# Two chained MLPs on one core: the last product's rows streamed over activations held as weights

## The chip, the cores and the metric

The kernel runs on one core of a Trainium2 chip. The metric is the device time of one execution in microseconds, and lower is better. Every time below was taken before the change.

## The reference

```python
B, S, D = 2, 4096, 192                # x; 8192 tokens in all, 8 heads of 24 features, 7 taps
w = softmax(weight_gen, axis=-1)      # (B, S, 8, 7), with 1e-9 added to the sum
x_unf = causal_windows(x, 7)          # each token and its 6 predecessors
x = einsum('bshk,bskhg->bshg', w, x_unf).reshape(8192, 192)

h = maximum(x @ w_in1, 0)             # w_in1 (192, 2048)
x = (h * h) @ w_out1                  # w_out1 (2048, 192)

h = x @ w_in2                         # w_in2 (192, 2048)
g = h * clip(h + 3, 0, 6) / 6
return g @ w_out2                     # w_out2 (2048, 192), result (8192, 192) float32
```

Four matrix products follow the small convolution: two for layer one, two for layer two. The change is to the last of them, `g @ w_out2`.

## The kernel before, in words

**Precision.** Every float32 operand of a product is split into a high part, rounded to the format fp32r, and a low part, the rest. A product is then high times high, plus high times low, plus low times high.

**Tokens.** The 8192 tokens are taken in 16 chunks of 512 (`CHUNKS`, `N`). Token rows are dealt so that partition p holds 64 consecutive rows, and a chunk is four of them in each of 128 partitions (`J = 4`).

**Steps.** The 2048 inner features are 16 tiles of 128, taken two at a time (`PAIR`), so that each layer of each chunk has 8 steps (`STEPS`) and the kernel has 256. In a step g TensorE makes the first product of step g into the bank pair `h_ps[:, s % 2]` and the second product of the step two before it (`LAG = 2`), from `hid_hi` and `hid_lo`, into `y1_ps` (layer one) or `y2_ps` (layer two). Between them ScalarE applies relu (L458), VectorE squares or gates (L820, L822), ScalarE rounds to the high part (L503) and VectorE takes the low part (L831), each over 128x1024 elements.

**Two halves of the array.** All these matmuls use 64 of the array's 128 rows: the upper half (partitions 64 to 127) and the lower half (0 to 63) run as two tiles side by side, on different PSUM banks. Each matmul has its own load of 128 weight columns, and the program alternates between the halves. One half of one step's first product is 9 matmuls of 512 columns (`hidden_part`, L1131). One half of one step's second product is 10 matmuls of 512 columns: six for the first 128 output features (`main_part`, L1141) and four for the other 64, whose high and low weights stand side by side in one 128-wide load (`rest_part`, L1149). So a step is 19 matmuls of 512 columns on each half. In each of them the output matrix is the weight and the 512 tokens are streamed, so the sums stand as features by tokens. `head`, `first_body` and `second_body` write out the order: in the first body the upper half makes the step's first product while the lower half finishes the second product; in the second body the roles are changed.

**The output.** Since the sums stand as features by tokens, ScalarE copies them out of PSUM with the factor 1/6 (`copy_o`, L552 and L553), VectorE adds the cross sum (`add_o`, L861) and turns 32x32 blocks (`turn_out`, L754 and L755), and the SP queue stores them in 32 small DMAs for each chunk (`store_turned`, L368 and L377). The last chunk is turned on TensorE instead (`turn_last_out`, L1291 and L1296) and stored by one DMA (L382).

**The last steps.** `last_bodies` and `output_sums` make the last chunk's sums; the last two steps' products use the full 128 rows of the array (L1253 to L1263).

**What sets the order.** Each engine's program is written out by hand, and engines wait on counting semaphores. TensorE waits, besides others, for `hi_done` and `lo_done` (the high and low inner activations of a step), and for its own `main_upper`, `main_lower`, `rest_upper` and `mm2_done`, which keep the two halves from adding into the same bank at once.

Of the kernel before, what the change touches and what calls it, by code (L numbers as in the profile page):

```python
# [18 lines left out]
def conv_mlp_kernel(nc: bass.Bass, x: bass.AP, weight_gen: bass.AP, w_in1: bass.AP, w_out1: bass.AP,  # L19
# [12 lines left out]
    P = 128  # L32
# [18 lines left out]
    HI_REST, LO_REST = slice(P, D), slice(D, D + REST)  # L51

# [52 lines left out]
    out_blocks = out.rearrange("(b t r) (f q) -> f t b r q", b=PBLOCKS, t=Q, q=Q)  # L105
# [5 lines left out]
    with ctx:  # L111
# [35 lines left out]
        o_main, o_rest, o_cross = outs[:, 0:N], outs[:, N:N + HALF], outs[0:REST, 2 * N:3 * N]  # L147
        out_sb = outs[:, 3 * N:3 * N + J * D].rearrange("p (a b d) -> p a b d", a=2, b=J // 2)
        out_main, out_rest = outs[:, 3 * N:4 * N], outs[:, 4 * N:4 * N + HALF]
# [63 lines left out]
        o_copied = sem("o_copied")  # L213
        o_added = sem("o_added")
# [3 lines left out]
        out_turned = sem("out_turned")  # L218
        last_turned = sem("last_turned")
# [20 lines left out]
        def low(n):  # L240

            layer, (kind, part, rest) = n // PIECES, PIECE[n % PIECES]
            hi, raw, _ = piece(n)
            if kind == "in":
                return [(win[layer][:, 2 * rest + 1, part * QC:(part + 1) * QC], raw, hi)]
            w = wout[layer][:, part * PT:(part + 1) * PT, :]
            return [(w[:, :, LO_MAIN], raw[:, :, 0:P], w[:, :, HI_MAIN]), (w[:, :, LO_REST], raw[:, :, P:D], w[:, :, HI_REST])]
# [71 lines left out]
        def _(sp):  # L319
# [31 lines left out]
            def store_turned(c):  # L351

                main = out_main.rearrange("p (n q) -> p n q", q=Q)
                rest = out_rest.rearrange("p (n q) -> p n q", q=Q)
                row_first = isinstance(c, int) and c < VECTOR

                def target(f, row):
                    return out_blocks[f][:, :, bass.ds(c * J + row, 1), :].rearrange("t b r q -> t b (r q)")

                def columns(blocks_of, row):  # L360
                    if row_first:
                        return blocks_of[:, row * PBLOCKS:(row + 1) * PBLOCKS, :]
                    return blocks_of.rearrange("p (b r) q -> p r b q", r=J)[:, row]

                sp.wait_ge(out_turned, 2 * c + 1)
                for f in range(P // Q):
                    for row in range(J):
                        sp.dma_start(target(f, row), columns(main[f * Q:(f + 1) * Q], row)).then_inc(out_stored, 16)  # L368
                sp.wait_ge(out_turned, 2 * c + 2)
                for half in range(2):  # L370
                    for f in range(REST // Q):
                        p0 = half * REST + f * Q
                        for n in range(J):

                            row, b0 = (half * JHALF + n // 2, n % 2 * 2) if row_first else (n, half * 2)
                            src = rest[p0:p0 + Q, 2 * n:2 * n + 2, :] if row_first else columns(rest[p0:p0 + Q], n)
                            sp.dma_start(target(P // Q + f, row)[:, b0:b0 + 2], src).then_inc(out_stored, 16)  # L377

            def store_last(c):
                sp.wait_ge(out_copied, 1)  # L380
                sp.wait_ge(out_scaled, 1)
                sp.dma_start(out_rows[:, bass.ds(c * (J * D), J * D)],  # L382
                             out_sb[:, :, :, :].rearrange("p a b d -> p (a b d)")).then_inc(out_stored, 16)
# [21 lines left out]
            def iteration(i):  # L405
                sp.wait_ge(exp_done, i + 2)
                load_gates(i + 2)
                move_blocks(i + 1)
                load_window(i + 2)
                store_turned(i - 2)  # L410
# [6 lines left out]
            for c in range(CHUNKS - 4, CHUNKS - 1):  # L417
                store_turned(c)
            store_last(CHUNKS - 1)
            sp.wait_ge(out_stored, STORES * (CHUNKS - 1) + 16)  # L420
# [19 lines left out]
        def _(act):  # L440
# [72 lines left out]
            def split_moved_hi(c, dst, free):  # L513
# [3 lines left out]
                act.activation(dst[:, 0, :], xs_main, ACT.Copy).then_inc(x1_hi, 1)  # L517
                act.wait_ge(x_rest_moved, 16 * (c - (VECTOR - 1)))
                act.activation(dst[REST:P, 3, :], xs_rest, ACT.Copy).then_inc(x1_hi, 1)
# [21 lines left out]
            def copy_o(c, steps, ps, final=0):  # L541

                act.wait_ge(mm2_done, steps)
                if not isinstance(c, int) or c >= 1:
                    act.wait_ge(out_turned, 2 * c)
                    act.wait_ge(out_stored, STORES * c)
                if final:
                    act.activation(row_major(o_cross), by_row(ps[REST:P, 1, :]), ACT.Copy).then_inc(o_copied, 1)
                    act.wait_ge(mm2_done, steps + 1)
                    act.activation(row_major(o_main), by_row(ps[:, 0, :]), ACT.Copy).then_inc(o_copied, 1)  # L550
                else:
                    act.activation(o_main[:, :], ps[:, 0, :], ACT.Copy, scale=1.0 / 6.0).then_inc(o_copied, 1)  # L552
                    act.activation(o_cross[:, :], ps[REST:P, 1, :], ACT.Copy, scale=1.0 / 6.0).then_inc(o_copied, 1)  # L553

            def copy_lower_out(c):

                act.wait_ge(last_turned, 1)
                act.wait_ge(out_stored, STORES * c)
                act.activation(out_sb[:, :, :, 0:REST].rearrange("p a b q -> p (a b) q"),
                               y2_ps[:, 0, 0:HALF].rearrange("p (j q) -> p j q", j=J), ACT.Copy, scale=1.0 / 6.0)  # L560
                act.activation(out_sb[:, 0, :, P:D], y2_ps[:, 0, HALF:2 * D].rearrange("p (b q) -> p b q", b=JHALF),
                               ACT.Copy, scale=1.0 / 6.0).then_inc(out_copied, 1)
# [79 lines left out]
            copy_o(CHUNKS - 1, g0 + STEPS, y1_ps, final=1)  # L642
            copy_lower_out(CHUNKS - 1)
# [3 lines left out]
        def _(dve):  # L647
# [103 lines left out]
            def turn_out(c):  # L751
                dve.wait_ge(o_copied, 2 * c + 2)
                dve.wait_ge(o_added, c + 1)
                dve.transpose(out_main, o_main).then_inc(out_turned, 1)  # L754
                dve.transpose(out_rest, o_rest).then_inc(out_turned, 1)  # L755

# [51 lines left out]
            def split_moved_lo(c, dst):  # L808
                dve.wait_ge(x1_hi, 2 * c + 2)
                dve.tensor_tensor(dst[:, 1, :], xs_main, dst[:, 0, :].bitcast(fp32), ALU.subtract).then_inc(x1_lo, 1)  # L810
                dve.wait_ge(x1_hi, 2 * c + 3)
                dve.tensor_tensor(dst[REST:P, 2, :], xs_rest, dst[REST:P, 3, :].bitcast(fp32),
# [39 lines left out]
            def add_o(c, ps, final=0):  # L852
                dve.wait_ge(o_copied, 2 * c + 2 - final)
                for half, rows in enumerate((slice(0, REST), slice(REST, P))):
                    if final:
                        js = slice(half * JHALF, (half + 1) * JHALF)
                        ins = dve.tensor_tensor(o_rest[rows, :].rearrange("p (j b i) -> p j b i", j=JHALF, i=Q),
                                                by_row(ps[0:REST, 1, :])[:, js], row_major(o_cross)[:, js], ALU.add)
                    else:
                        cols = slice(half * HALF, (half + 1) * HALF)  # L860
                        ins = dve.scalar_tensor_tensor(out=o_rest[rows, :], in0=ps[0:REST, 1, cols], scalar=1.0 / 6.0,  # L861
                                                       in1=o_cross[:, cols], op0=ALU.mult, op1=ALU.add)
                ins.then_inc(o_added, 1)

            def iteration(i, prep, last):
                g0 = first_step(i) if isinstance(i, int) else dve.snap(i * (2 * STEPS) - STEPS)
                for s in range(2 * STEPS):
# [11 lines left out]
                    if s == 12:  # L879
                        turn_out(i - 2)  # L880
# [3 lines left out]
                    if s == 2:  # L884
                        add_o(i - 2, y2_ps)
# [69 lines left out]
            for s in range(STEPS):  # L955
                gate(g0 + s, 1, s % 2)
                hidden_lo(g0 + s, s % 2, own=s - (STEPS - 2) if s >= STEPS - 2 else None)
                if s == 2:
                    add_o(CHUNKS - 2, y2_ps)
                if s == 3:  # L960
                    turn_out(CHUNKS - 2)
            add_o(CHUNKS - 1, y1_ps, final=1)
            dve.wait_ge(last_turned, 1)
            dve.wait_ge(out_stored, STORES * (CHUNKS - 1))
            dve.tensor_scalar(out_sb[:, :, :, REST:P].rearrange("p a b q -> p (a b) q"),
                              y2_ps[:, 1, 0:HALF].rearrange("p (j q) -> p j q", j=J), 1.0 / 6.0, None, ALU.mult)
            dve.tensor_scalar(out_sb[:, 1, :, P:D], y2_ps[:, 1, HALF:2 * D].rearrange("p (b q) -> p b q", b=JHALF), 1.0 / 6.0,
                              None, ALU.mult).then_inc(out_scaled, 1)
# [3 lines left out]
        def _(pe):  # L972
# [179 lines left out]

            def head(g, late, rest_of):

# [263 lines left out]
```

## Time and profile before

| what | value |
|---|---|
| median of 3 runs | 1126.98 us (1126.95 to 1127.29) |
| profiled execution, span of core 0 | 1125.2 us |
| TensorE matmuls busy | 1119.4 us (99%), 9940 instructions |
| TensorE weight loads busy | 1082.5 us (96%), 9940 instructions |
| VectorE busy | 906.8 us (81%) |
| ScalarE busy | 668.8 us (59%) |
| granted TensorE clock | 1.00 throughout |
| DMA packets | 79302, of which 56172 are under 512 B |

The profiled execution is a run of its own; its own time is known by its span alone, from the first instruction to the last, and the runs' times hold what lies around such a span as well. Matmuls are pipelined and their rows overlap: a row's duration is longer than the distance to the next matmul of the same half, so how fast TensorE works is read from the distances between starts.

### The profile page before, as it was taken

The page shows a single profiled execution, that of the slowest core. Times are in us where ns is not written, and L with a number is a line of the kernel's source. Part 1 is how long each engine was busy: PE and PEld are TensorE (multiplying, and loading weights), DVE is VectorE, ACT ScalarE, POOL GpSimd, SP SyncE. Part 2 cuts the span into 40 slices and gives each one's busy share as a digit, 9 for nine tenths or more (in the row PEclk, how much of TensorE's full clock was granted, in tenths as well). Part 3 has the DMA queues.
Part 4 walks back from the last instruction along what each step waited for, and adds up shares of the span by engine and source line. Part 5 has one row for each costly group of instructions (what it writes and reads, how often), then busy time and mean ns, then how long its engine had stood idle before and what let it go on. Part 6 is the DMA issues. An engine that isn't in the chain of part 4 may idle for free.

```text
span 1125.2 us, 25509 instructions
## 1 busy us (share of the span) xinstructions
PE 1119.4 (99%) x9940; PEld 1082.5 (96%) x9940; DVE 906.8 (81%) x985; ACT 668.8 (59%) x747; POOL 3.1 (0%) x10
## 2 busy tenths in 40 slices
PE   9999999999999999999999999999999999999998
PEld 8998999999999999999999999999999999999997
DVE  8788796987969789697887978879698797976665
ACT  7986556565565655645556555555655556456554
POOL 1000000000000000000000000000000000000000
PEclk9999999999999999999999999999999999999999
DMA  7221002020110201103020020200202002010001
GB/s 214 86 66 36 6 16 63 4 74 7 30 48 3 75 6 57 25 0 77 4 66 15 0 77 4 70 11 8 69 4 73 8 17 59 0 40 4 1 16 29
DMA packets 79302, 41.28 MB, mean 37 GB/s; under 512 B 56172, under 2 KB 72300, under 8 KB 79272
## 3 DMA queue, kind: packets, MB, share of 16 engines
q1 hardware_dynamic: 79144, 40.64, 13.9%
q8 instruction: 21, 0.34, 0.1%
q10 hardware_dynamic: 128, 0.22, 0.1%
q14 instruction: 9, 0.07, 0.0%
HBM read 29.42 MB, written 11.40 MB: 36 GB/s over the span
## 4 chain that ended last, share of the span: by engine, by line
PE 99%; DVE 0%; DMA 0%; ACT 0%; issue 0%; DVEq 0%
PE h_ps L1131 46%; PE y_ps L1141 31%; PE y_ps L1149 21%; PE h_ps L988 0%; DMA wraw<-in_weight_gen_dram 0%; PE y_ps L1099 0%; PE y_ps L988 0%; PE y_ps L1272 0%; PE h_ps L1099 0%; PE y_ps L1253 0%; DVE prod L721 0%; PE y_ps L1254 0%; PE y_ps L1259 0%; PE y_ps L1256 0%; PE h_ps L1089 0%
## 5 line engine op out<-in xcount | busy, mean ns | idle before, releaser
L1131 PE MATMUL h_ps<-xt,win 64*128 64x512 f32 x4552 | 1026.4, 386 | 0.0
L1131 PEld LDWEIGHTS h_ps<-xt,win 64*128 64x128 f32 x4552 | 801.3, 184 | 14.9
L1141 PE MATMUL y_ps<-hid_hi,wout 64*128 64x512 f32 x2032 | 542.5, 386 | 0.0
L503 ACT ACTIVATE hid_hi<-hid 128x1024 fp32r<-128x1024 f32 x240 | 254.7, 1061 | 328.9 <-DVE hid L822 166.0
L831 DVE TENSOR_TENSOR hid_lo<-hid,hid_hi 128x1024 fp32r<-128x1024 f32 x253 | 309.5, 1223 | 147.6 <-ACT hid_hi L503 141.5
L1141 PEld LDWEIGHTS y_ps<-hid_hi,wout 64*128 64x128 f32 x2032 | 373.3, 184 | 7.1 <-PE y_ps L1141 0.3
L1141 PE MATMUL y_ps<-hid_lo,wout 64*128 64x512 f32 x1016 | 311.6, 386 | 0.0
L1149 PE MATMUL y_ps<-hid_hi,wout 64*128 64x512 f32 x1016 | 311.4, 386 | 0.0
L1149 PE MATMUL y_ps<-hid_lo,wout 64*128 64x512 f32 x1016 | 311.3, 386 | 0.0
L1141 PEld LDWEIGHTS y_ps<-hid_lo,wout 64*128 64x128 f32 x1016 | 186.8, 184 | 4.0 <-DVE hid_lo L806 0.3
L1149 PEld LDWEIGHTS y_ps<-hid_hi,wout 64*128 64x128 f32 x1016 | 186.9, 184 | 3.7 <-PE y_ps L1149 0.3
L1149 PEld LDWEIGHTS y_ps<-hid_lo,wout 64*128 64x128 f32 x1016 | 186.9, 184 | 3.4
L822 DVE SCALAR_TENSOR_TENSOR hid<-hid,h_ps 128x1024 f32<-128x1024 f32 x128 | 155.8, 1217 | 31.4 <-ACT hid L458 31.1
L458 ACT ACTIVATE hid<-h_ps,three 128x1024 f32<-128x1024 f32 x128 | 142.8, 1115 | 62.7 <-PE h_ps L1131 60.4
L458 ACT ACTIVATE hid<-h_ps 128x1024 f32<-128x1024 f32 x126 | 129.0, 1024 | 45.2 <-PE h_ps L1131 44.8
L820 DVE TENSOR_TENSOR hid<-hid 128x1024 f32<-128x1024 f32 x114 | 139.5, 1223 | 18.4 <-ACT hid L458 17.5
L657 DVE TENSOR_TENSOR acc<-acc,prod 128x768 f32<-128x768 f32 x84 | 80.1, 954 | 0.6
L670 DVE TENSOR_TENSOR prod<-xwin,prob 128x768 f32<-128x768 f32 x84 | 80.0, 953 | 0.0
L670 DVE TENSOR_TENSOR acc<-xwin,prob 128x768 f32<-128x768 f32 x14 | 13.4, 958 | 1.6
L500 ACT ACTIVATE hid_hi<-hid 128x1024 fp32r<-128x1024 f32 x13 | 13.8, 1058 | 1.2
L492 ACT ACTIVATE hid<-hid 128x1024 f32<-128x1024 f32 x13 | 13.8, 1062 | 0.4
L840 DVE TENSOR_TENSOR xt<-y_main,xt 128x512 fp32r<-128x512 f32 x16 | 11.0, 685 | 2.4 <-ACT xt L534 2.4
(116 smaller groups left out, 358.1 us busy)
## 6 DMA issues: line engine op xcount, KB each, us to landing
xwin<-in_x_dram SPq DMA_DIRECT2D x14, 960.0 KB, 5.9
by_feature<-stage SPq DMA_DIRECT2D x52, 96.0 KB, 2.0
out_dram<-outs SPq DMA_DIRECT2D x240, 16.0 KB, 1.5
out_dram<-outs SPq DMA_DIRECT2D x240, 8.0 KB, 1.4
stage<-by_feature SPq DMA_DIRECT2D x13, 256.0 KB, 3.0
stage<-in_moe_w_out_dram SPq DMA_DIRECT2D x8, 384.0 KB, 3.6
stage<-in_moe_w_in_dram SPq DMA_DIRECT2D x8, 256.0 KB, 3.7
stage<-in_moe_w_in_dram SPq DMA_DIRECT2D x16, 128.0 KB, 3.7
```

Source lines behind the costliest of these rows:

```text
L458: act.activation(hid[:, slot], sums_of(g, slot), ACT.Relu, **bias).then_inc(relu_done, 1)
L492: act.activation(hid[:, slot], hid[:, slot], ACT.Square).then_inc(squared, 1)
L500: act.activation(hi, hid[:, slot], ACT.Copy).then_inc(hi_done, 1)
L503: act.activation(hi, hid[:, slot], ACT.Copy).then_inc(hi_done, 1)
L657: done(dve.tensor_tensor(acc[:, :], acc[:, :], prod[:, k % 2, :], ALU.add))
L670: done(dve.tensor_tensor(dst.rearrange("p (n g) -> p n g", g=GROUP), src.rearrange("p (n g) -> p n g", g=GROUP), probs_of[:, :, tap:tap + ...
L820: dve.tensor_tensor(h, h, h, ALU.mult).then_inc(gated, 1)
L822: dve.scalar_tensor_tensor(out=hid[:, slot], in0=hid[:, slot], scalar=6.0, in1=h_ps[:, slot], op0=ALU.min, op1=ALU.mult).then_inc(gated, 1)
L831: dve.tensor_tensor(lo, hid[:, slot], hi.bitcast(fp32), ALU.subtract).then_inc(lo_done, 1)
L1131: return pe.matmul(h_ps[:, s % 2, t, :], win[layer][r, wn, cols], src[r, xn, :], start=bool(rows) and n in (0, SHORT), stop=not rows and n ...
L1141: return pe.matmul(ps[:, 0, :], wout[layer][r, tile, w_cols], src, start=bool(rows) and s == 0 and n == 0, stop=not rows and s == STEPS - ...
L1149: return pe.matmul(ps[:, 1, :], wout[layer][r, PAIR * s + t, HI_LO_REST], src, start=bool(rows) and s == 0 and n == 0, stop=not rows and s ...
```

## The change

In layer two's second product the roles of the operands are exchanged. A block of 128 tokens of `hid_hi` or `hid_lo` is the weight, and 192 columns of the output matrix, either the high or the low part of its rows, are streamed. The sums stand as tokens by features: two token blocks of 192 features in each of the two banks of `ps`. Layer one's second product is left as it was.

One half of a step's second product becomes 24 units (`UNITS`): for each of 2 tiles and 4 token blocks, high activations by high weights, high by low, and low by high. Each has its own weight load. `LOWER_BY` and `UPPER_BY` say how many units stand behind each of the other half's nine `hidden_part` matmuls, two or three.

The output's way gets shorter: one ScalarE copy (`copy_o`) and one VectorE copy (`scale_o`) with the factor 1/6, each of 128x384, and one DMA of 384 KB for each chunk (`store_rows`), two DMAs for the last chunk. `add_o`, `turn_out`, `turn_last_out` and `copy_lower_out` go. Because a sum's row is now a token, the tokens of chunks 3 and later are brought into row order where layer one's input is split (`split_moved_hi`, `split_moved_lo`), through views with runs of 32 elements. The full-array `output_sums` is left for the last step alone; the step before it is made by halves in `last_bodies`. TensorE waits for `out_copied` and `out_scaled` where it waited for `o_added`.

```diff
+    ROW_HI, ROW_LO = slice(0, D), slice(D, 2 * D)
-    STORES = 16 * J * (P // Q + 2 * (REST // Q))
+    STORES = 16
+    def high_units(bank, t):
+        return [(bank, t, j, False, cols) for cols in (ROW_HI, ROW_LO) for j in range(JHALF)]
+    def low_units(bank):
+        return [(bank, t, j, True, ROW_HI) for t in range(PAIR) for j in range(JHALF)]
+    UNITS = (high_units(0, 0) + high_units(0, 1) + high_units(1, 0) + low_units(0) + high_units(1, 1) + low_units(1))
+    FIRST_OF = (0, 8)
+    LOW_OF = 12
+    LAST_OF = (15, 23)
+    LOWER_BY = (3, 5, 7, 10, 12, 15, 17, 20, 22, 24)
+    UPPER_BY = (0, 3, 5, 8, 10, 13, 15, 17, 20, 22)
...
-                act.activation(dst[:, 0, :], xs_main, ACT.Copy).then_inc(x1_hi, 1)
+                act.activation(row_major(dst[:, 0, :]), by_row(xs_main), ACT.Copy).then_inc(x1_hi, 1)
...
+                act.activation(out_sb[:, 0, :], ps[:, 0, 0:JHALF * D], ACT.Copy, scale=1.0 / 6.0).then_inc(out_copied, 1)
...
+                dve.tensor_scalar(out_sb[:, 1, :], ps[:, 1, 0:JHALF * D], 1.0 / 6.0, None, ALU.mult).then_inc(out_scaled, 1)
...
+            def row_part(rows, n, s, ps):
+                bank, t, j, is_low, cols = UNITS[n]
+                r = slice(0, P) if rows is None else ROWS_OF[rows]
+                src = (hid_lo if is_low else hid_hi)[:, s % 2]
+                if ps is y1_ps and s >= STEPS - 2:
+                    src = (last_lo if is_low else last_hi)[s - (STEPS - 2)]
+                tokens = slice((bank * JHALF + j) * P, (bank * JHALF + j + 1) * P)
+                return pe.matmul(ps[:, bank, j * D:(j + 1) * D], src[r, t, tokens], wout[1][r, PAIR * s + t, cols],
+                                 start=rows == 1 and s == 0 and n in FIRST_OF, stop=rows != 1 and s == STEPS - 1 and n in LAST_OF,
+                                 skip_group_check=True, tile_position=(r.start, 0))
+            def row_head(g, s, ps):
+                pe.wait_ge(main_upper, g - LAG)
+                row_part(0, 0, s, ps)
+                row_part(1, 22, s, ps)
+                row_part(0, 1, s, ps)
+                row_part(1, 23, s, ps).then_inc(rest_upper, 1)
+            def row_first_body(g, inn, s, ps, gated_before):
+                sums_free(g, gated_before)
+                row_part(0, 2, s, ps)
+                for n in range(2 * SHORT + 1):
+                    up = hidden_part(1, n, *inn)
+                    ...
+                    for m in range(LOWER_BY[n], LOWER_BY[n + 1]):
+                        if m == FIRST_OF[1]:
+                            pe.wait_ge(rest_upper, g - LAG)
+                        low = row_part(0, m, s, ps)
+                        ...
+                low.then_inc(mm2_done, 1)
+            def row_second_body(g, inn, s, ps):
+                for n in range(2 * SHORT + 1):
+                    ...
+                    low = hidden_part(0, n, *inn)
+                    for m in range(UPPER_BY[n], UPPER_BY[n + 1]):
+                        if m == FIRST_OF[0]:
+                            pe.wait_ge(hi_done, g - LAG + 1)
+                            pe.wait_ge(main_lower, g - LAG)
+                        if m == FIRST_OF[1]:
+                            pe.wait_ge(mm2_done, g - LAG)
+                        if m == LOW_OF:
+                            pe.wait_ge(lo_done, g - LAG + 1)
+                        up = row_part(1, m, s, ps)
+                        ...
+                low.then_inc(mm1_done, 1)
```

## Rows read from the trace of the kernel before

**Rows 1.** The page: busy time by engine, and the chain that ended last.
```profile
PE 1119.4 (99%) x9940; PEld 1082.5 (96%) x9940; DVE 906.8 (81%) x985; ACT 668.8 (59%) x747; POOL 3.1 (0%) x10
...
PE 99%; DVE 0%; DMA 0%; ACT 0%; issue 0%; DVEq 0%
```
**Rows 2.** A group by line (busy us, mean ns, idle), and a window with TensorE's clock.
```profile
L1131 PE MATMUL h_ps<-xt,win 64*128 64x512 f32 x4552 | 1026.4, 386 | 0.0
...
500.00:700.00 200.00, 200.00 (x1768) 194.72 (x1766) 164.89 (x178) 115.85 (x127) 0.00 (x0) 1.00 0.14 34
```
**Rows 3.** Timeline of matmuls in mid-kernel: start us, duration us, engine, line.
```profile
700.04 0.39 PE L1131 MATMUL h_ps<-xt,win 64*128 64x512 f32 x1
700.08 0.39 PE L1141 MATMUL y_ps<-hid_hi,wout 64*128 64x512 f32 x1
700.27 0.39 PE L1131 MATMUL h_ps<-xt,win 64*128 64x512 f32 x1
...
700.95 0.39 PE L1131 MATMUL h_ps<-xt,win 64*128 64x512 f32 x1
```
**Rows 4.** Timeline of weight loads in the same stretch.
```profile
700.04 0.18 PEld L1131 LDWEIGHTS h_ps<-xt,win 64*128 64x128 f32 x1
700.08 0.18 PEld L1141 LDWEIGHTS y_ps<-hid_hi,wout 64*128 64x128 f32 x1
700.27 0.18 PEld L1131 LDWEIGHTS h_ps<-xt,win 64*128 64x128 f32 x1
```
**Rows 5.** Timeline of ScalarE's relu of layer two, one a step.
```profile
704.13 1.12 ACT L458 ACTIVATE hid<-h_ps,three 128x1024 f32<-128x1024 f32 x1 [0.90 <-PE h_ps L1131]
708.43 1.12 ACT L458 ACTIVATE hid<-h_ps,three 128x1024 f32<-128x1024 f32 x1 [0.84 <-PE h_ps L1131]
```
**Rows 6.** Timeline of loads near the end, full array, after a pause.
```profile
1115.38 0.19 PEld L1253 LDWEIGHTS y_ps<-win,wout 128*128 128x128 f32 x1 [0.35 <-issue]
1115.49 0.19 PEld L1254 LDWEIGHTS y_ps<-win,wout 128*128 128x128 f32 x1
```
**Rows 7.** Timeline of the matmul that belongs to the first of these loads.
```profile
1115.39 0.50 PE L1253 MATMUL y_ps<-win,wout 128*128 128x512 f32 x1
```
**Rows 8.** Timeline after a pause on both halves: four loads, four matmuls.
```profile
12.64 0.30 PEld L988 LDWEIGHTS h_ps<-xt,win 64*128 64x128 f32 x4 [0.27 <-ACT xt L473]
...
12.65 0.72 PE L988 MATMUL h_ps<-xt,win 64*128 64x512 f32 x4
```
**Rows 9.** Short float32 matmuls at the start: one timeline stretch, and the loads' group.
```profile
8.84 0.44 PE L1089 MATMUL h_ps<-ident 64*128 64x128 f32 x4
...
L1089 PEld LDWEIGHTS h_ps<-ident 64*128 64x128 f32 x16 | 1.2, 191 | 0.0
...
8.78 0.31 PEld L1089 LDWEIGHTS h_ps<-ident 64*128 64x128 f32 x4
```
**Rows 10.** Waits: engine and line, what it waited for, us in total, times, longest.
```profile
ACT hid_hi L503 <- DVE hid L822: 166.0, 124, 2.4
DVE hid_lo L831 <- ACT hid_hi L503: 141.5, 158, 1.6
```
**Rows 11.** Groups by line, the output's way out of PSUM and copies of like size.
```profile
L861 DVE SCALAR_TENSOR_TENSOR outs<-y_ps,outs 64x256 f32<-64x256 f32 x30 | 12.4, 413 | 0.2
L754 DVE STREAM_TRANSPOSE outs<-outs 128x512 f32<-128x512 f32 x15 | 10.6, 704 | 0.0
L721 DVE TENSOR_TENSOR prod<-outs,prob 128x384 f32<-128x384 f32 x2 | 1.0, 554 | 0.0
L552 ACT ACTIVATE outs<-y_ps 128x512 f32<-128x512 f32 x15 | 8.9, 591 | 0.0
```
**Rows 12.** Timeline of the end: last bodies, last sums, turning, last store.
```profile
1110.99 0.42 PE L1131 MATMUL h_ps<-xt,win 64*128 64x512 f32 x2
...
1119.60 0.61 PE L1263 MATMUL y_ps<-win,wout 128*128 128x512 f32 x2
...
1122.48 0.35 SPq L382 DMA_DIRECT2D out_dram<-outs  x1
```

More of the change, by code:

```diff
@@ L93, in conv_mlp_kernel @@
     MOST, FEW = [(1, 49)], [(49, PB)]
-    STORES = 16 * J * (P // Q + 2 * (REST // Q))
+    STORES = 16
[7 more added lines that the diff above has]
+    LAST_OF = (15, 23)
+    BANK = [[n for n, unit in enumerate(UNITS) if unit[0] == bank] for bank in range(2)]
+    LOWER_BY = (3, 5, 7, 10, 12, 15, 17, 20, 22, 24)
+    UPPER_BY = (0, 3, 5, 8, 10, 13, 15, 17, 20, 22)
     def first_step(i):
@@ L349, in move_blocks @@
                 sp.dma_start(xs_rest, by_feature[P:D, :]).then_inc(x_rest_moved, 16)
[L351 to L377, printed above, removed]
@@ L850, in split_x2_lo, with scale_o @@
                 split_x2_rest_lo(c, dst)
[L852 to L863, printed above, removed]
+            def scale_o(c, steps, ps):
+                dve.wait_ge(mm2_done, steps)
+                if not isinstance(c, int) or c >= 1:
+                    dve.wait_ge(out_stored, STORES * c)
+                dve.tensor_scalar(out_sb[:, 1, :], ps[:, 1, 0:JHALF * D], 1.0 / 6.0, None, ALU.mult).then_inc(out_scaled, 1)
             def iteration(i, prep, last):
@@ L1212, in rest_unit @@
                                      xt[0][REST:P, 3, :], start=False, stop=stop, tile_position=(REST, 0))
-                for n, unit in enumerate((0, 1, 2, 5, 6, 7)):
-                    if n in (0, 3):
-                        pe.wait_ge(first_upper, 2 * (g - LAG) + 1 + n // 3)
+                done, s, ps = g - LAG, out[1], out[2]
+                units = {0: (0, 1, 2), 1: (3, 4), 2: (5, 6, 7), 5: (12, 13), 6: (14, 15)}
+                for unit in units:
+                    if unit in (0, 5):
+                        pe.wait_ge(first_upper, 2 * done + 1 + unit // 5)
@@ new lines, in last_bodies @@
+                hidden_part(0, 8, *inn).then_inc(last_lower, 1)
+                pe.wait_ge(mm2_done, done)
+                for n in range(len(BANK[0])):
+                    up = row_part(1, BANK[1][n], s, ps)
+                    if n == 0:
+                        pe.wait_ge(main_upper, done + 1)
+                    low = row_part(0, BANK[0][n], s, ps)
+                up.then_inc(rest_upper, 1)
+                low.then_inc(main_lower, 1)
+                for n in range(len(BANK[0])):
+                    if n == 0:
+                        pe.wait_ge(rest_upper, done + 1)
+                    low = row_part(0, BANK[1][n], s, ps)
+                    if n == 0:
+                        pe.wait_ge(hi_done, done + 2)
+                        pe.wait_ge(main_lower, done + 1)
+                    if BANK[0][n] == LOW_OF:
+                        pe.wait_ge(lo_done, done + 2)
+                    up = row_part(1, BANK[0][n], s + 1, ps)
@@ new lines, in last_bodies @@
+                low.then_inc(mm2_done, 1)
+                up.then_inc(main_upper, 1)
+                for n in range(len(BANK[0])):
+                    if n == 0:
+                        pe.wait_ge(mm2_done, done + 1)
+                    up = row_part(1, BANK[1][n], s + 1, ps)
+                    if n == 0:
+                        pe.wait_ge(main_upper, done + 2)
+                    low = row_part(0, BANK[0][n], s + 1, ps)
+                up.then_inc(rest_upper, 1)
+                low.then_inc(main_lower, 1)
@@ new lines, in last_bodies, with output_sums @@
+                pe.wait_ge(rest_upper, done + 2)
+                for n in BANK[1]:
+                    low = row_part(0, n, s + 1, ps)
+                low.then_inc(mm2_done, 1)
+            def output_sums(g, s, ps):
+                pe.wait_ge(hi_done, g + 1)
+                for bank in range(2):
+                    for n in BANK[bank]:
+                        if not UNITS[n][3]:
+                            row_part(None, n, s, ps)
+                pe.wait_ge(lo_done, g + 1)
+                for bank, whole_sum in enumerate((main_lower, mm2_done)):
+                    for n in BANK[bank]:
+                        if UNITS[n][3]:
+                            ins = row_part(None, n, s, ps)
+                    ins.then_inc(whole_sum, 1)
```

159 lines of the change are left out of this document (51 added, 108 removed).

## The prediction

> **What bounds the kernel now.** I read the page's busy shares and its chain first: TensorE is busy for 99% of the span and is 99% of the chain that ended last, VectorE 81%, ScalarE 59% [rows 1]. The groups by line show no idle time before TensorE's matmuls [rows 2]. So only what TensorE's own stream costs can move the time, beside the few microseconds at the end. What that stream costs is a matter of distances between starts, so the timeline comes next. On one half of the array the first product's matmuls start at 700.04, 700.27 and, four matmuls on from the first, 700.95: 0.91 us for four, 0.227 us each; the other half runs the same distance, 0.04 us later [rows 3]. A step is 19 of these, 19 x 0.227 = 4.31 us, and relu, which comes once a step, shows 708.43 - 704.13 = 4.30 us [rows 5]. 512 columns at the granted 2.4 GHz are 213 ns, so 14 ns of each distance is not streaming.
>
> Then the weight loads: on each half a load starts just when a matmul of that half starts (700.04 and 700.04, 700.27 and 700.27; 700.08 on the other half), that is, the load for the following matmul, behind the stream of the present one [rows 3, 4]. Never is more than one load ahead. With 512 columns there is room: the stream lasts 0.227 us. What the load takes by itself shows only where TensorE had paused and nothing hid it. At 1115.38 a load starts, its matmul's row lasts 0.50 us where later ones last 0.39, and the following load starts at 1115.49, 0.11 us behind the first, because the first matmul could begin only then [rows 6, 7]. At 12.64 both halves do so at once: four loads take 0.30 us with 0.19 for the last, so the second pair starts 0.11 us after the first, and four matmuls take 0.72 us, which is 0.39 for the last plus one distance of 0.227 plus 0.11 for the load [rows 8]. A load of 128 weight columns therefore holds its half for about 0.11 us, on 64 rows and on 128 alike, and the two halves' loads don't hinder each other.
>
> The Trainium skill, "TensorE: Matmul & The Clock Gate", section LDWEIGHTS, says that a load costs its columns over 1.2 GHz whatever the rows, 107 ns for 128, by an estimate from its figure. The trace agrees with 0.11 us, and the rule speaks against this change, which has 24 loads where there were 10.
>
> **The change part by part.** *Streamed columns.* One half's share of a step's second product goes from 10 x 512 = 5120 to 24 x 192 = 4608 columns. At 2.4 GHz 512 columns fewer are 0.21 us of a step, which would be the gain if nothing but columns counted.
>
> *Distance of two units.* 192 columns stream in 80 ns, with the 14 ns from above 94 ns. But the load of the next unit starts only when the present one starts and takes 0.11 us, so the distance is that of the load. No row before shows a 192-column matmul. The nearest is the 128-column one of [rows 9]: per half two loads, four in all in 0.31 us with 0.19 for the last, so 0.12 us apart. From below, 0.105 us is what rounding leaves of the 0.11; from above, the 14 ns may stand on top of the load, 0.125 us. I take 0.110 us, the value of [rows 6 to 8], since these are loads of the same format.
>
> *One step.* In the first body the lower half has 22 units against 9 matmuls of 512 of the upper half: 22 x 0.110 = 2.42 us against 9 x 0.227 = 2.04 us. TensorE starts matmuls in the written order, so the upper half waits for the units between its own. In the second body it is the same with the halves exchanged. The head has two units for each half, 0.22 us. That would be 46 distances; about one is saved where the roles change, as that half's first load is already there. 45 x 0.110 = 4.95 us against 4.31, so +0.64 us a step. Of the 128 steps of layer two's second product (16 chunks of 8) two are in the written-out end: 126 x 0.64 = +81 us. Before, the 9 and the 10 matmuls of the halves were all of one length and nobody waited; now each body is as long as its row of units. With 0.105 a step is 4.73 us and the change +53 us; with 0.125 it is 5.63 us and +166 us.
>
> *Waits of TensorE.* The activations come from relu, gate, high and low part. ScalarE waits 166 us in all for the gate and 105 us for TensorE, VectorE 141 us for the high part [rows 10]: these engines wait for each other within a step and lose nothing when it gets longer. `hi_done` is needed a step and a half after the sums are there. The waits of the halves for each other's bank lie at least seven units, 0.7 us, behind what they wait for. Nothing there, unless a step stayed at 4.3 us, where it would still be the cover of before. The output waits are on copies made a dozen steps earlier.
>
> *The output's way.* For each chunk ScalarE's two copies of 0.59 us become one, VectorE's two adds of 0.41 us and transposes of 0.70 and 0.40 us become one copy near 0.55 us, which is the time of a 128x384 operation [rows 11]. The 32 DMAs become one. All of this lies beside TensorE's stream and is worth nothing in the middle. The split of layer one's input through strided views is four operations a chunk of 0.6 to 0.7 us [rows 11]; even at twice the time they are 2.6 us in 70, ahead of a use at the next chunk: nothing.
>
> *The end.* Before: from 1110.99, where the last step's second body begins, to the last sum at 1119.60 + 0.61 - 0.22 = 1119.99 is 9.0 us, and the way out until 1125.2 is 5.2 us [rows 12]. After: the last body has five 512-column matmuls with 12 units among them, two intervals of three units at 0.33 and three at 0.227, 1.34 us; then two distances of 0.227, 0.45 us; then 48 distances of units (three runs of 12 pairs, one of 12 alone), 5.28 us; then 24 units on the full array, 2.64 us: 9.7 us. The way out is 0.1 for the semaphore, a copy of about 0.55 and what stood behind the copies before, 1125.2 - 1122.45 = 2.75: 3.4 us. 13.1 against 14.2: -1.1 us.
>
> *Sum.* 1125.2 + 81 - 1.1 = 1205.1 us of span. The median stands 1.8 us above the profiled span: 1207 us.
>
> **The rivals.**
>
> *The loads stay hidden.* If a load can begin before the present unit does, or its 0.11 us is mostly latency, units go by their stream: 94 ns. Then 22 units are 2.06 us against the other half's 2.04, a step is 2 x 2.06 + 2 x 0.094 = 4.31 us less the change of roles, some 4.29, and the kernel saves 126 x 0.02 = 2.5 us, at the end 72 x 0.016 + 0.1 us more, 1.1 + 1.3 = 2.4: 1122 us. This is the case on the other side, and it decides at a load of 94 ns. If the 14 ns belonged to columns and not to matmuls, units would take 85 ns, and the nine matmuls of 512 columns would bound each body: 2 x 2.04 + 0.17 = 4.25 us, -7.6 us and -3 at the end, 1116 us. The saving is small even so, because the two halves' bodies are matched and 9 x 0.227 stays. For it: the rows of loads overlap matmuls throughout, and busy loads of 96% hurt nobody today. Against it: a load never starts ahead of the present matmul in [rows 4].
>
> The Trainium skill's same page, section Back-to-back issue gap, gives N/2.4 + 2.5 ns, 82 ns for 192 columns by an estimate, which takes no account of the load; this rule would lead to the second of these times. The trace disagrees for 512 columns: 227 ns against 216.
>
> *The load pays the 14 ns too.* 0.125 us a unit: 1127 + 166 = 1293 us. For it: 0.12 in [rows 9]. Against: in [rows 6] the whole from load to load is 0.11.
>
> *Loads share one path.* Were only one load possible at a time, a step would take 66 x 0.108 = 7.1 us: +2.8 x 126, 1480 us. Against it: [rows 8], where two run at once.
>
> *Narrow streams lose their rate.* The plain f32 matmuls of [rows 9] show two records for each written matmul, so 0.24 us for 128 columns. If fp32r fell to such a rate below some width, a unit would take 0.35 us and a step 45 x 0.35 = 16 us: beyond 2500 us. Nothing in the trace shows fp32r under 512 columns, so it can't be excluded.
>
> **How the numbers follow.** The forecast with 0.105 to 0.12 us holds 0.71, the load with 14 ns on top 0.09, hidden loads 0.15 (0.12 of it faster by over 0.2%, 0.03 within), the shared path 0.03, the lost rate 0.02. 0.2% is about what a measurement of this kernel can tell from no change. The range 1180 to 1295 us takes in the first two, 0.80; its ends are 1127 + 53 and the 0.125 case. Faster 0.12, same 0.03, slower 0.85.
>
> **What would show it.** Right: layer two's relu 4.9 to 5.0 us apart in steps 11 to 15 and 0 to 2 of a chunk and 4.3 in the others; units of one half 0.11 us apart, loads starting with the matmuls; no idle time but between the 512-column matmuls of the other half; both other engines less busy in share. Wrong: units 0.08 to 0.095 us apart (loads hidden), a step near 4.3; or idle TensorE ahead of `hi_done` or of its own semaphores; or steps of 7 us and more.

## The result, and the profile after

| | before | after |
|---|---|---|
| median | 1127.03 us | 1180.37 us (1180.22 to 1180.86) |
| ratio to before | 1 | 1.0473, 95% interval 1.0458 to 1.0488 |
| profiled span | 1125.2 us | 1179.1 us |
| TensorE matmuls | 9940 | 13508 |
| DMA packets | 79302 | 27850 |

The change costs 53.3 us. The page of the changed kernel, the line of busy times and the head of the chain, against [rows 1]:

```profile
PE 1174.4 (100%) x13508; PEld 1157.1 (98%) x13508; DVE 890.3 (76%) x933; ACT 662.0 (56%) x729; POOL 3.1 (0%) x10
...
PE 99%; DMA 0%; DVE 0%; SPq 0%; issue 0%; ACT 0%
```

TensorE is still the whole chain, and the other engines have less to do in a longer time. A group by line of the changed kernel (count, then busy us, mean ns, idle before) shows the new units at L1115 with next to no idle time before them:

```profile
L1115 PE MATMUL y_ps<-wout,hid_hi 64*128 64x192 f32 x4032 | 505.5, 269 | 0.1
```

Where the time went is read from relu once more, whose rows stand one step apart [rows 5]. The timeline of ScalarE, changed kernel, relu's rows alone, first two rows inside layer two's second product and then two around layer one's:

```profile
681.53 1.12 ACT L450 ACTIVATE hid<-h_ps,three 128x1024 f32<-128x1024 f32 x1 [1.02 <-PE h_ps L1085]
686.27 1.12 ACT L450 ACTIVATE hid<-h_ps,three 128x1024 f32<-128x1024 f32 x1 [1.02 <-PE h_ps L1085]
...
709.93 1.03 ACT L450 ACTIVATE hid<-h_ps 128x1024 f32<-128x1024 f32 x1 [0.86 <-PE h_ps L1085]
714.24 1.03 ACT L450 ACTIVATE hid<-h_ps 128x1024 f32<-128x1024 f32 x1 [0.24 <-PE h_ps L1085]
```

Steps with the new units take 4.74 us, the others 4.31 us as before. 0.43 us for each of 126 steps is 54 us: this is the whole loss.

Inside such a step, the timeline of weight loads of the changed kernel:

```profile
696.09 0.30 PEld L1115 LDWEIGHTS y_ps<-wout,hid_hi 64*128 64x128 f32 x2
696.22 0.18 PEld L1085 LDWEIGHTS h_ps<-xt,win 64*128 64x128 f32 x1
696.32 0.30 PEld L1115 LDWEIGHTS y_ps<-wout,hid_hi 64*128 64x128 f32 x2
696.45 0.18 PEld L1085 LDWEIGHTS h_ps<-xt,win 64*128 64x128 f32 x1
696.54 0.30 PEld L1115 LDWEIGHTS y_ps<-wout,hid_hi 64*128 64x128 f32 x2
696.68 0.18 PEld L1085 LDWEIGHTS h_ps<-xt,win 64*128 64x128 f32 x1
696.76 0.19 PEld L1115 LDWEIGHTS y_ps<-wout,hid_lo 64*128 64x128 f32 x1
```

From 696.09 to 696.76 there are six unit loads on the lower half, 0.112 us each (the first and the last of each merged pair lie 0.30 - 0.19 = 0.11 apart). On the upper half the 512-column matmuls' loads come 0.23 us apart, at the pace of [rows 4], and not at that of the units between them. That is the part that I had not expected.

The same shows where the roles change, here from the first to the second body (timeline of matmuls, changed kernel):

```profile
697.81 0.39 PE L1085 MATMUL h_ps<-xt,win 64*128 64x512 f32 x1
697.86 0.39 PE L1115 MATMUL y_ps<-wout,hid_lo 64*128 64x192 f32 x2
698.04 0.25 PE L1115 MATMUL y_ps<-wout,hid_hi 64*128 64x192 f32 x1
698.08 0.27 PE L1115 MATMUL y_ps<-wout,hid_lo 64*128 64x192 f32 x1
698.13 0.27 PE L1115 MATMUL y_ps<-wout,hid_hi 64*128 64x192 f32 x1
698.19 0.41 PE L1085 MATMUL h_ps<-xt,win 64*128 64x512 f32 x1
```

The upper half's last 512-column matmul starts at 697.81 and its first unit at 698.04, one distance of 0.227 us later, without a pause. As the program is written, this unit stands behind the lower half's last two units (697.97 and 698.08) and its first 512-column matmul (698.19). Its load starts at 697.86, before any of these three has begun.

The end, changed kernel:

```profile
1174.32 1.84 PE L1115 MATMUL y_ps<-wout,win 128*128 128x192 f32 x15
...
1175.74 0.49 ACT L538 ACTIVATE outs<-y_ps 128x384 f32<-128x384 f32 x1 [5.11 <-PE y_ps L1115]
1176.19 0.56 DVE L827 TENSOR_SCALAR outs<-y_ps 128x384 f32<-128x384 f32 x1 [4.30 <-PE y_ps L1115]
1176.26 0.85 SPq L374 DMA_DIRECT2D out_dram<-outs  x2
```

The last sum's row ends at 1174.32 + 1.84 = 1176.16 and the span at 1179.1: 2.9 us of way out. Counted alike, from the end of the last row at 1119.60 + 0.61 = 1120.21, it was 5.0 us before [rows 12].

### The profile page after: what moved, and what is told of

The parts are those of the page before. It is cut to its first block, busy times and chain, and to the rows that moved or that the text cites. A ratio compares the mean times of both kernels' runs of the same rounds, so it can differ in the third digit from the quotient of the medians.

```text
span 1179.1 us, 31535 instructions
## 1 busy us (share of the span) xinstructions
PE 1174.4 (100%) x13508; PEld 1157.1 (98%) x13508; DVE 890.3 (76%) x933; ACT 662.0 (56%) x729; POOL 3.1 (0%) x10
## 2 busy tenths in 40 slices
DMA packets 27850, 41.34 MB, mean 35 GB/s; under 512 B 2668, under 2 KB 19052, under 8 KB 27816
## 4 chain that ended last, share of the span: by engine, by line
PE 99%; DMA 0%; DVE 0%; SPq 0%; issue 0%; ACT 0%
PE h_ps L1085 43%; PE y_ps L1115 30%; PE y_ps L1095 15%; PE y_ps L1103 10%; PE h_ps L942 0%; DMA outs<-in_x_dram 0%; PE y_ps L1053 0%; PE y_ps L942 0%; PE y_ps L1307 0%; PE h_ps L1053 0%; DVE prod L696 0%; PE h_ps L1043 0%; DVE outs L827 0%; PE y_ps L1319 0%; SPq L330 0%
## 5 line engine op out<-in xcount | busy, mean ns | idle before, releaser
L1085 PE MATMUL h_ps<-xt,win 64*128 64x512 f32 x4552 | 1104.4, 388 | 0.0
L1085 PEld LDWEIGHTS h_ps<-xt,win 64*128 64x128 f32 x4552 | 819.4, 184 | 6.2
L1115 PE MATMUL y_ps<-wout,hid_hi 64*128 64x192 f32 x4032 | 505.5, 269 | 0.1
L1115 PEld LDWEIGHTS y_ps<-wout,hid_hi 64*128 64x128 f32 x4032 | 481.6, 187 | 0.4 <-PE y_ps L1115 0.2
L1115 PE MATMUL y_ps<-wout,hid_lo 64*128 64x192 f32 x2016 | 303.9, 270 | 0.0
L1095 PE MATMUL y_ps<-hid_hi,wout 64*128 64x512 f32 x1024 | 273.6, 387 | 0.0
L1115 PEld LDWEIGHTS y_ps<-wout,hid_lo 64*128 64x128 f32 x2016 | 263.1, 188 | 0.0
L792 DVE SCALAR_TENSOR_TENSOR hid<-hid,h_ps 128x1024 f32<-128x1024 f32 x128 | 155.9, 1218 | 53.3 <-ACT hid L450 53.3
L1095 PEld LDWEIGHTS y_ps<-hid_hi,wout 64*128 64x128 f32 x1024 | 187.9, 184 | 3.1
L1095 PE MATMUL y_ps<-hid_lo,wout 64*128 64x512 f32 x512 | 157.2, 387 | 0.0
L1103 PE MATMUL y_ps<-hid_hi,wout 64*128 64x512 f32 x512 | 156.9, 386 | 0.0
L1103 PE MATMUL y_ps<-hid_lo,wout 64*128 64x512 f32 x512 | 156.9, 386 | 0.0
L1095 PEld LDWEIGHTS y_ps<-hid_lo,wout 64*128 64x128 f32 x512 | 94.1, 184 | 2.0 <-DVE hid_lo L775 0.3
L1103 PEld LDWEIGHTS y_ps<-hid_hi,wout 64*128 64x128 f32 x512 | 94.2, 184 | 1.6
L1103 PEld LDWEIGHTS y_ps<-hid_lo,wout 64*128 64x128 f32 x512 | 94.2, 184 | 1.5
```

The costliest lines, as they stand in the source:

```text
L792: dve.scalar_tensor_tensor(out=hid[:, slot], in0=hid[:, slot], scalar=6.0, in1=h_ps[:, slot], op0=ALU.min, op1=ALU.mult).then_inc(gated, 1)
L1085: return pe.matmul(h_ps[:, s % 2, t, :], win[layer][r, wn, cols], src[r, xn, :], start=bool(rows) and n in (0, SHORT), stop=not rows and n ...
L1095: return pe.matmul(ps[:, 0, :], wout[layer][r, tile, w_cols], src, start=bool(rows) and s == 0 and n == 0, stop=not rows and s == STEPS - ...
L1103: return pe.matmul(ps[:, 1, :], wout[layer][r, PAIR * s + t, HI_LO_REST], src, start=bool(rows) and s == 0 and n == 0, stop=not rows and s ...
L1115: return pe.matmul(ps[:, bank, j * D:(j + 1) * D], src[r, t, tokens], wout[1][r, PAIR * s + t, cols], start=rows == 1 and s == 0 and n in ...
```

## Experiments

All runs are timed in three rounds beside the kernel before (1126.96 to 1127.04 us). Step lengths are read from relu rows as above, unit distances from the loads of L1115.

### Smaller loads

```diff
-                tokens = slice((bank * JHALF + j) * P, (bank * JHALF + j + 1) * P)
-                return pe.matmul(ps[:, bank, j * D:(j + 1) * D], ...
+                tokens = slice((bank * JHALF + j) * P, (bank * JHALF + j) * P + 96)
+                return pe.matmul(ps[0:96, bank, j * D:(j + 1) * D], ...
```

> Only 96 of each block's 128 tokens are taken as weights in layer two's second product, so a quarter of its sums is left out; units, their order and the 192 streamed columns stay. Theory A (a unit lasts as long as the following unit's load, 0.112 us for 128 columns; a half's step is the sum of its own matmuls, 24 x 0.112 + 9 x 0.227 = 4.72 us): the load falls to 0.084 us, the stream with its 14 ns, 0.094 us, takes over, a step is 24 x 0.094 + 2.04 = 4.29 us, and the kernel takes 1180 - 126 x 0.43 = 1126 us. Theory B (a 192-column matmul costs 80 ns plus 32 ns whatever its load): nothing changes, 1180 us.

1116.88 us, ratio 0.9909 (0.9893 to 0.9926). Theory B falls: with the same streams and three quarters of each load the whole loss is gone. The timeline of loads has them 0.09 us apart (two in 0.25 with 0.16 for the last, three in 0.34):

```profile
710.07 0.25 PEld L1115 LDWEIGHTS y_ps<-wout,hid_hi 64*96 64x96 f32 x2
...
710.25 0.34 PEld L1115 LDWEIGHTS y_ps<-wout,hid_hi 64*96 64x96 f32 x3
...
710.51 0.25 PEld L1115 LDWEIGHTS y_ps<-wout,hid_hi 64*96 64x96 f32 x2
...
710.70 0.34 PEld L1115 LDWEIGHTS y_ps<-wout,hid_hi 64*96 64x96 f32 x3
```

From 710.07 to 710.70 are seven units, 0.090 us each. I had put 0.094; the 0.004 are 24 x 0.004 x 126 = 12 us, and 9 us is by how much the time lies under the 1126 expected. With the load the matmul too gets narrower here, and this edit can't part the two. That it is the load is read from the places where a load stood alone and took 0.11 us [rows 6 to 8].

### Shorter streams

```diff
-                return pe.matmul(ps[:, bank, j * D:(j + 1) * D], src[r, t, tokens], wout[1][r, PAIR * s + t, cols],
+                return pe.matmul(ps[:, bank, j * D:j * D + P], src[r, t, tokens], wout[1][r, PAIR * s + t, slice(cols.start, cols.start + P)],
```

> Each unit streams 128 columns of the output matrix instead of 192, so a third of the output's features is left out; loads and order stay. Theory A (the load bounds a unit): no change, 1180 us, units 0.112 us apart. Theory B (80 ns of stream plus 32 ns): a unit lasts 53 + 32 = 85 ns, a step 24 x 0.085 + 2.04 = 4.08 us, and the kernel takes 1180 - 126 x 0.65 = 1098 us.

1185.48 us, ratio 1.0517 (1.0499 to 1.0534): a third of the stream less brings nothing, it is even 5 us slower than the change. The loads stay 0.11 us apart, two in 0.30 with 0.19 for the last:

```profile
695.91 0.30 PEld L1115 LDWEIGHTS y_ps<-wout,hid_hi 64*128 64x128 f32 x2
```

With the run before, this settles that the load bounds a unit. The 5 us are steps of 4.77 us against 4.74. The timeline of matmuls shows where they lie:

```profile
679.08 0.39 PE L1085 MATMUL h_ps<-xt,win 64*128 64x512 f32 x1
...
680.70 0.39 PE L1085 MATMUL h_ps<-xt,win 64*128 64x512 f32 x1
```

These are seven distances of 512-column matmuls beside the units, 0.231 us each, where the changed kernel has 0.227 (1.59 us for seven, from 696.22 to 697.81). Nine in a step are 0.04 us, and 126 times that 5 us. Why they stand further apart here is open.

### Longer streams

```diff
-                return pe.matmul(ps[:, bank, j * D:(j + 1) * D], src[r, t, tokens], wout[1][r, PAIR * s + t, cols],
+                return pe.matmul(ps[:, bank, j * HALF:(j + 1) * HALF], src[r, t, tokens], wout[1][r, PAIR * s + t, slice(min(cols.start, 2 * D - HALF), min(cols.start, 2 * D - HALF) + HALF)],
```

> Each unit streams 256 columns instead of 192 and adds 64 columns that belong to no sum, so the output isn't the reference's; loads and order stay. Theory A with 14 ns for each matmul beside its stream: 107 + 14 = 0.120 us passes the load's 0.112, a step is 24 x 0.120 + 2.04 = 4.92 us, 1180 + 126 x 0.19 = 1204 us. If the 14 ns belonged to columns (0.227 us for 512), a unit would be 0.113 us and the time 1183 us. Theory B (stream plus 32 ns): 0.139 us a unit, a step 5.38 us, 1262 us.

1207.99 us, ratio 1.0716 (1.0698 to 1.0734), against 1204 expected, with steps of 4.94 us:

```profile
690.85 1.12 ACT L450 ACTIVATE hid<-h_ps,three 128x1024 f32<-128x1024 f32 x1 [0.92 <-PE h_ps L1085]
695.79 1.12 ACT L450 ACTIVATE hid<-h_ps,three 128x1024 f32<-128x1024 f32 x1 [1.15 <-PE h_ps L1085]
```

At 256 columns the stream and what a matmul costs beside it, about 0.12 us, just pass the load. So the two costs cross between 192 and 256 columns.

### Fewer loads for the same columns

```diff
-        return [(bank, t, j, False, cols) for cols in (ROW_HI, ROW_LO) for j in range(JHALF)]
+        return [(bank, t, j, False, slice(0, 2 * D)) for j in range(JHALF)]
...
-    LOWER_BY = (3, 5, 7, 10, 12, 15, 17, 20, 22, 24)
-    UPPER_BY = (0, 3, 5, 8, 10, 13, 15, 17, 20, 22)
+    LOWER_BY = (3, 4, 6, 7, 9, 10, 12, 13, 15, 16)
+    UPPER_BY = (0, 2, 3, 5, 6, 8, 9, 11, 12, 14)
...
+                elif not is_low:
+                    dst = ps[:, bank, j * REST:j * REST + 2 * D]
```

> The same columns are streamed with fewer loads: high activations take the high and the low part of the output matrix's rows in one stream of 384 columns, so a step has 16 loads for each half instead of 24. The 384 sums run into columns that overlap with the next block's, so the output isn't the reference's; only the time counts. Theory A: a pair of units costs 160 + 14 = 0.174 us for the long one and 0.112 for the short one, a step is 8 x 0.286 + 2.04 = 4.33 us, 1180 - 126 x 0.40 = 1129 us. Theory B (stream plus 32 ns): 8 x (0.192 + 0.112) + 2.04 = 4.47 us, 1180 - 126 x 0.26 = 1147 us. Were it the streamed columns that cost the time, nothing would change, 1180 us.

1137.20 us, ratio 1.0089 (1.0072 to 1.0106). Of the 53 us, 43 are gone with a third of the loads, the streamed columns being the same. It lies between theory A (1129) and B (1147), and does not tell them apart by itself, with steps of 4.38 to 4.40 us where A had 4.33:

```profile
723.89 1.12 ACT L450 ACTIVATE hid<-h_ps,three 128x1024 f32<-128x1024 f32 x1 [0.32 <-PE h_ps L1085]
728.27 1.12 ACT L450 ACTIVATE hid<-h_ps,three 128x1024 f32<-128x1024 f32 x1 [0.56 <-PE h_ps L1085]
```

Of the remaining 0.06 us of a step some 0.04 lie again in the 512-column matmuls, which stand 0.231 us apart (1.39 us for six, from 724.34 to 725.73); their cause and the rest are open. Even in this form, which has no room in the two banks for real sums, the exchanged roles would not beat the kernel before.

### Small loads and short streams together

```diff
-                tokens = slice((bank * JHALF + j) * P, (bank * JHALF + j + 1) * P)
-                return pe.matmul(ps[:, bank, j * D:(j + 1) * D], ...
+                tokens = slice((bank * JHALF + j) * P, (bank * JHALF + j) * P + 96)
+                return pe.matmul(ps[0:96, bank, j * D:j * D + P], ...
```

> Weights of 96 tokens and streams of 128 columns together, so a quarter of the tokens and a third of the features are left out. The 96-column weights with 192 streamed columns gave units 0.090 us apart, which can be 0.080 of stream plus 0.010, or the load. If it is the load (0.090 for 96 columns, 0.112 for 128): units stay 0.090 us apart and the time stays at 1117 us. If it was the stream, the load of 96 columns is 0.112 x 96/128 = 0.084: 24 x 0.006 x 126 = 18 us less, 1099 us.

1103.88 us, ratio 0.9794 (0.9778 to 0.9811): nearer to 1099 than to 1117. So with 96-column loads and 192 streamed columns the stream was the bound, at 0.090 us, 0.080 and 0.010 beside it. Now loads stand 0.085 us apart (two in 0.25 with 0.16 for the last, and three in 0.33):

```profile
710.06 0.16 PEld L1115 LDWEIGHTS y_ps<-wout,hid_hi 64*96 64x96 f32 x1
...
710.14 0.33 PEld L1115 LDWEIGHTS y_ps<-wout,hid_hi 64*96 64x96 f32 x3
```

0.085 for 96 columns and 0.112 for 128 are the same price for each column. The 5 us over 1099 are of the size that the shorter streams cost above; here too the 512-column matmuls stand further apart than 0.227 us (0.93 us for four, from 711.08 to 712.01).

### The written order of the two halves

```diff
-    LOWER_BY = (3, 5, 7, 10, 12, 15, 17, 20, 22, 24)
-    UPPER_BY = (0, 3, 5, 8, 10, 13, 15, 17, 20, 22)
+    LOWER_BY = (3, 3, 3, 10, 10, 10, 17, 17, 17, 24)
+    UPPER_BY = (0, 0, 0, 8, 8, 8, 15, 15, 15, 22)
```

> The changed kernel with its units in three lumps of 7 or 8 behind every third 512-column matmul of the other half, instead of 2 or 3 behind each; instructions and output are the same. Theory A (each half goes through its own matmuls without regard to the other's place in the written order, as far as a look-ahead of some 20 instructions goes): 24 x 0.112 + 9 x 0.227 = 4.72 us a step as before, 1180 us within 10. Theory C (matmuls of the two halves start in the written order, as my prediction had it): a lump cycle is two distances of 0.227 with the other half idle and then 7.3 units, 0.454 + 0.82 = 1.27 us, six cycles and a head 7.8 us a step, 1180 + 126 x 3.1 = 1570 us.

1228.46 us, ratio 1.0900 (1.0882 to 1.0918). Both theories miss: 1180 and 1570. Theory C, a strict written order, would have made a step of 7.8 us and falls. But theory A without a limit falls too: a step now takes 5.11 us (relu at 700.81 and at 705.92), not 4.74.

Both halves now stand idle at a change of roles. The timeline of matmuls from the first to the second body:

```profile
703.04 0.39 PE L1085 MATMUL h_ps<-xt,win 64*128 64x512 f32 x1
...
703.18 0.61 PE L1115 MATMUL y_ps<-wout,hid_lo 64*128 64x192 f32 x4
703.52 0.35 PE L1115 MATMUL y_ps<-wout,hid_hi 64*128 64x192 f32 x1
703.63 0.42 PE L1085 MATMUL h_ps<-xt,win 64*128 64x512 f32 x1
```

The upper half's last 512-column matmul is through at 703.04 + 0.227 = 703.27. Its first unit is written behind all the lower half's units and behind three of its 512-column matmuls. Its load starts at 703.52, when the last of those units begins (703.18 + 0.61 - 0.27) and only the three matmuls are left, and the unit follows one load later, at 703.63. So the half was idle for 0.36 us, which is what a step gained, 5.11 - 4.74 = 0.37. To measure how far it can get, one table was changed on one side:

```diff
-    UPPER_BY = (0, 3, 5, 8, 10, 13, 15, 17, 20, 22)
+    UPPER_BY = (0, 0, 0, 0, 0, 13, 15, 17, 20, 22)
```

> The changed kernel with one table changed: in the second body the upper half's first 13 units are written behind the lower half's fifth 512-column matmul instead of 3 behind the first, 2 behind the second and so on; the first body, all instructions and the output are the same. In the trace of the changed kernel the upper half's first unit was loaded while three earlier-written matmuls of the lower half had not begun. If such a look-ahead has no limit: 1180 us. If it reaches over three matmuls (theory A, amended): the unit must wait until the lower half's second 512-column matmul has begun, some 0.5 us later than now, a step is 5.2 us, 1180 + 126 x 0.5 = 1245 us. If matmuls start in the written order (theory C): it waits for the fifth, 1.09 us later than now, 1180 + 126 x 1.09 = 1317 us.

1230.47 us, ratio 1.0917 (1.0899 to 1.0936), between the 1180 of an unlimited look-ahead and the 1317 of none, and nearest to 1245. The timeline of matmuls of this run at the change of roles:

```profile
699.51 0.39 PE L1085 MATMUL h_ps<-xt,win 64*128 64x512 f32 x1
...
699.75 0.64 PE L1085 MATMUL h_ps<-xt,win 64*128 64x512 f32 x2
700.01 0.46 PE L1115 MATMUL y_ps<-wout,hid_hi 64*128 64x192 f32 x2
700.23 0.39 PE L1085 MATMUL h_ps<-xt,win 64*128 64x512 f32 x1
700.32 0.39 PE L1115 MATMUL y_ps<-wout,hid_hi 64*128 64x192 f32 x2
700.46 0.39 PE L1085 MATMUL h_ps<-xt,win 64*128 64x512 f32 x1
700.54 0.38 PE L1115 MATMUL y_ps<-wout,hid_hi 64*128 64x192 f32 x2
700.70 0.39 PE L1085 MATMUL h_ps<-xt,win 64*128 64x512 f32 x1
700.76 0.60 PE L1115 MATMUL y_ps<-wout,hid_hi 64*128 64x192 f32 x4
701.11 0.50 PE L1085 MATMUL h_ps<-xt,win 64*128 64x512 f32 x1
```

The upper half's last 512-column matmul starts at 699.51 and is through by 699.74. Its first unit, written behind five 512-column matmuls of the lower half, comes at 700.01, just when the second of these five starts (the merged row's last starts at 699.75 + 0.64 - 0.39 = 700.00), and ahead of the ones at 700.23, 700.46 and 700.70. So it went past three matmuls that had not begun, and no more. The unit's load was not hidden either, for it started only then. The timeline of weight loads has

```profile
700.01 0.41 PEld L1115 LDWEIGHTS y_ps<-wout,hid_hi 64*128 64x128 f32 x3
```

The second of these three loads starts at 700.12, and a load starts with the matmul before it, so the unit itself began at 700.12. The half was idle from 699.74 to 700.12, 0.38 us, where the changed kernel has no pause at this place. This is the 0.39 us that a step gained over 4.74. The lower half shows the same limit: its sixth 512-column matmul, written behind all 13 units, starts at 701.11, just behind the tenth of them (the last of the four from 700.76 on), with three left.

### Is the output's way off the critical path?

```diff
+                spare = 4 * N + HALF
+                dve.transpose(outs[:, spare:spare + HALF], o_rest)
+                dve.transpose(outs[:, spare + HALF:spare + HALF + P], o_main[:, 0:P])
                 dve.transpose(out_main, o_main).then_inc(out_turned, 1)
```

> The kernel before with two more 32x32-block transposes on VectorE in each chunk's output (128x256 and 128x128 elements, together about 0.65 us), written to a spare place. If the output's way off TensorE costs nothing, as my prediction had it: 1127 us, no change. If VectorE's output work delays the low parts and with them TensorE: up to 15 x 0.65 = +10 us, 1137 us, and then part of the change's output work was a gain that the units' cost hides.

1127.03 us, ratio 1.0001 (0.9991 to 1.0011). VectorE has 0.71 us more for each chunk (two groups of this run, count, busy and mean):

```profile
L755 DVE STREAM_TRANSPOSE outs<-outs 128x256 f32<-128x256 f32 x15 | 6.6, 437 | 0.0
...
L756 DVE STREAM_TRANSPOSE outs<-outs 128x128 f32<-128x128 f32 x15 | 4.0, 269 | 0.0
```

10.6 us of VectorE work are worth nothing here, so this much of VectorE's output work is hidden. The 32 DMAs and ScalarE's copies were not tried alone; that they were hidden too is argued from TensorE's unbroken chain.

## Why the prediction was right, and where its centre was off

The direction held, and so did the main mechanism, that weight loads bound the units; how the two halves share a step did not. 1180.4 us lies at the lower end of the range of 1180 to 1295, against a centre of 1207. The measured loss is 53 us where the sum had 80.

1. *A unit lasts as long as a load.* Right, and shown by the runs with smaller loads, shorter streams and both. The value was 0.110 us, measured 0.112.
2. *The written order binds the halves.* This step failed: "TensorE starts matmuls in the written order, so the upper half waits for the units between its own". It gave a step of 45 unit distances, 4.95 us. The halves in fact keep their own pace, and at a change of roles the half that is ready goes ahead of the other, past up to three matmuls. Each half then takes just the sum of its own matmuls, 24 x 0.112 + 9 x 0.227 = 4.73 us, and 4.74 was measured. With the true load and the rule of the prediction a step would have been 45 x 0.112 = 5.04 us and the loss 92 us; so the term was sized 0.64 us instead of 0.43. That 45 x 0.105, my lower bound, also gives 4.73 is an accident: the distance is 0.112. It is also what made the lower end of my range 1180, 0.4 us under the measured time, so that the time lies inside the range is luck; what held is the direction and the price of the load.
3. *Other work beside TensorE.* Right as far as tried: more VectorE work on the output changed nothing. ScalarE's copy of 128x384 took 485 ns and VectorE's 550 where I had 0.55 for both:

```profile
L538 ACT ACTIVATE outs<-y_ps 128x384 f32<-128x384 f32 x16 | 7.8, 485 | 5.1 <-PE y_ps L1115 5.1
L827 DVE TENSOR_SCALAR outs<-y_ps 128x384 f32<-128x384 f32 x16 | 8.8, 550 | 4.3 <-PE y_ps L1115 4.3
L509 ACT ACTIVATE xt<-stage 128x512 fp32r<-128x512 f32 x13 | 8.0, 615 | 0.0
```

   The last of these rows is the split through strided views: 615 ns, what it was without them. I had allowed twice that.
4. *The end.* The sum had -1.1 us. The last step's second body starts at 1165.25 and the span ends 13.9 us later; before it was 14.2. Counted as in the prediction, from 0.22 us before the end of the last row, the way out was 3.2 us against my 3.4, but the sums before it took 10.7 against my 9.7. The gain is some 0.3 us. What my sum left out is that TensorE waits for its own last unit where the runs of units change banks. Timelines of the changed kernel, the start of the last body and the loads at the first such change:

```profile
1165.25 0.41 PE L1085 MATMUL h_ps<-xt,win 64*128 64x512 f32 x1
...
1168.43 0.18 PEld L1115 LDWEIGHTS y_ps<-wout,hid_hi 64*128 64x128 f32 x1 [0.23 <-PE y_ps L1115]
```

   No load starts in these 0.23 us, and the load that follows is not hidden. There are three such changes between the runs of units; by an estimate from this one, 0.23 us and a load of 0.11 each, they cost 1 us in all.

5. *The rivals.* The hidden loads are refuted by the 128-column streams, a shared path and a lost rate by steps of 4.74 us, and the 14 ns on top of the load by the distance of 0.112.

The written-order step is what would have told 1180 from 1207. Nothing in the trace before could show it, since there all matmuls had one length and the halves never drifted apart; a hidden assumption should have been a bound of the sum: with each half on its own, 24 x 0.110 + 2.04 = 4.68 us, the loss would have been 47 us.

## What to carry to other kernels

Before exchanging weights and streamed operand, count the loads: a matmul lasts for the longer of its own stream and the next load on its rows. Here 24 loads at 0.112 us cost 2.68 us where 10 streams of 512 columns cost 2.27, though a tenth of the columns was saved; a unit had to be under 2.27 / 24 = 0.094 us to pay. And where two halves of the array work side by side, sum each half by itself first, and only then ask how far the written order lets one get ahead of the other; here it was three matmuls.

## What the hardware showed that was not expected

- A unit of one half was loaded ahead of three earlier-written matmuls of the other half that had not begun (697.86 in the changed kernel), and in the run with late units it did not go before just three were left. The lumped run stops at three as well, at 703.52. Further than three was not seen. At the other change of roles in the lumped run the lower half did not get ahead like this: its last 512-column matmul starts at 700.39, its first unit's load at 700.86, behind every earlier-written matmul. This unit also waits for `main_upper`, but the matmul that raises it starts at 700.17 and its row ends at 700.44, so why it came so late is open.
- A weight load costs by its columns alone: 0.112 us for 128 and 0.085 for 96, each on 64 rows, and about 0.11 on 128 rows [rows 6].
- What a matmul costs beside its stream is not one number: 0.010 us at 192 columns (96-column loads), about 0.013 at 256 and at 512 [rows 3], and 0.018 at 512 beside the 128-column units and beside the 384-column ones (0.231 us from start to start).
